# Seven block products (Strassen's scheme) instead of eight in the second layer of an attention and two-layer kernel, in tiles of 768 tokens

## What is computed

```python
def _moe_ref(x, w_in, w_out, s, b):
    h = x @ w_in
    r = np.maximum(h, 0.0)
    g = s * (r * r) + b
    return (g @ w_out).astype(np.float32)

def _moe2_ref(x, w_in, w_out):
    h = x @ w_in
    g = h - np.tanh(h)
    return (g @ w_out).astype(np.float32)
```

## Time and profile before

| | |
|---|---|
| median of 3 runs | 911.38 us (910.88 to 911.38) |
| span of the profiled execution (its own time isn't listed beside it) | 909.3 us |
| TensorE busy | 895.9 us, 6100 matmuls |
| VectorE busy | 501.7 us |
| ScalarE busy | 425.0 us |
| GpSimd busy | 279.4 us |
| mean granted TensorE clock | 0.998 |

### The profile page before, as it was taken

The page is one execution under the profiler, slowest core; times in us unless marked ns, Lnnn a source line. Parts: engine busy times, 40 slices in busy tenths (PEclk is TensorE's granted clock), DMA queues, the critical chain, the costliest instruction groups (busy, mean ns, idle before and its releaser), DMA issues.

```text
span 909.3 us, 15682 instructions
## 1 busy us (share of the span) xinstructions
PE 895.9 (99%) x6100; PEld 846.0 (93%) x6100; DVE 501.7 (55%) x635; ACT 425.0 (47%) x1060; POOL 279.4 (31%) x280
## 2 busy tenths in 40 slices
PE   6999999999999999999999999999999999999998
PEld 6789999999999999999999999999999999999997
DVE  5658599989999999982104632323323323322322
ACT  2899585566546754446457722322323223222221
POOL 6568474966497653534222000000000000000000
PEclk9999999999999999999999999999999999999999
DMA  8962453343344223002225400200200100100101
GB/s 217 274 236 55 127 146 85 91 121 85 97 114 115 62 61 78 19 2 65 66 77 181 165 1 1 70 1 1 70 1 22 49 1 1 35 1 1 35 1 35
DMA packets 48333, 65.15 MB, mean 72 GB/s; under 512 B 18246, under 2 KB 30084, under 8 KB 48260
## 3 DMA queue, kind: packets, MB, share of 16 engines
q1 hardware_dynamic: 45865, 62.42, 24.8%
q10 hardware_dynamic: 2395, 1.74, 0.8%
HBM read 54.71 MB, written 9.44 MB: 71 GB/s over the span
## 4 chain that ended last, share of the span: by engine, by line
PE 95%; ACT 2%; DMA 1%; DVE 1%; issue 1%; SPq 1%; ACTq 0%; DVEq 0%
PE acc L1918 22%; PE hid L1937 22%; PE hid L1890 21%; PE acc L1955 21%; PE pa L1848 1%; PE pa L1815 1%; DMA dkey<-in_k_dram 1%; PE pa L1832 1%; PE pa L1690 1%; PE pa L1861 1%; PE acc L1967 0%; PE hid L1898 0%; SPq L867 0%; PE hid L1796 0%; PE pa L1753 0%
## 5 line engine op out<-in xcount | busy, mean ns | idle before, releaser
L1057 POOL TENSOR_TENSOR gl<-relu,gh 128x288 fp32r<-128x288 f32 x128 | 128.6, 1008 | 185.9 <-PE acc L1918 129.5
L1361 DVE TENSOR_TENSOR gdif<-hid,tanh 128x384 f32<-128x384 f32 x96 | 53.5, 558 | 184.4 <-ACT tanh L1638 184.2
L1918 PE MATMUL acc<-gh,wbh 128*128 128x288 f32 (+1 forms) x512 | 154.6, 302 | 0.0
L1890 PE MATMUL hid<-xh,wah 128*128 128x288 f32 x512 | 153.5, 301 | 0.3 <-ACT relu L1597 0.2
L1918 PE MATMUL acc<-gl,wbh 128*128 128x288 f32 (+1 forms) x512 | 151.5, 296 | 0.0
L1918 PE MATMUL acc<-gh,wbl 128*128 128x288 f32 (+1 forms) x512 | 151.1, 295 | 0.0
L1890 PE MATMUL hid<-xh,wal 128*128 128x288 f32 x512 | 150.4, 295 | 0.0
L1890 PE MATMUL hid<-xl,wah 128*128 128x288 f32 x484 | 142.0, 294 | 0.0
L1638 ACT ACTIVATE tanh<-hid 128x384 f32<-128x384 f32 x96 | 47.2, 491 | 186.3 <-PE hid L1937 186.3
L1937 PE MATMUL hid<-x2h,wal 128*128 128x384 f32 x384 | 129.0, 336 | 0.0
L1937 PE MATMUL hid<-x2h,wah 128*128 128x384 f32 x384 | 128.9, 336 | 0.0
(11 more groups left out here) (162 smaller groups left out, 1549.9 us busy)
## 6 DMA issues: line engine op xcount, KB each, us to landing
wa_raw<-in_moe_w_in_dram SPq DMA_DIRECT2D x8, 1024.0 KB, 7.8
wb_raw<-in_moe_w_out_dram SPq DMA_DIRECT2D x8, 1024.0 KB, 6.3
kl<-in_k_dram SPq DMA_DIRECT2D x23, 240.0 KB
vl<-in_v_dram SPq DMA_DIRECT2D x23, 240.0 KB
...
x2raw<-x2T SPq DMA_DIRECT2D x6, 768.0 KB, 4.5
...
```

Source lines behind the costliest of these rows:

```text
L1057: g.tensor_tensor(out=gl[:, turn % LRING1, 0:NS], in0=relu[:, f % 2, :], in1=gh[:, turn % GRING1, 0:NS].bitcast(F32), op=ALU.subtract).the ...
L1361: ve.tensor_tensor(gdif[:, f % 2, :], hid[:, f % 2, 0:N2], tanh[:, f % 2, :], ALU.subtract).then_inc(s_dif, 1)
L1890: one = pe.matmul(dst, w[:, d, cols], x[:, j % XRING, d, :], start=i == 0, stop=i == 3 * KT - 1)
L1918: one = pe.matmul(acc[:, d, n], w[:, f, cols], g[:, turn % ring, n], start=(f == 0 and p == 0), stop=(f == FT - 1 and p == 2))
```

## The change

The tile becomes 768 tokens, in two halves of 384, and there are three. The hidden blocks are taken in pairs (`QUADS` = 8). For a pair, w_in is four blocks (two halves of the 512 inputs by two hidden blocks) and x2 is four blocks (two halves of the inputs by two halves of the tokens), and the four blocks of the hidden result are made from seven products of sums of these, not from eight plain ones (Winograd's form of Strassen's scheme). One pair in one tile is a step; there are 24. In a step:

- `product` p1, p6, p2, p7, p4, p5, p3: six matmuls of 384 columns each. p1 and p2 add up in bank 0 of `hid`, p7 and p4 in bank 1, p5 and p3 in bank 0.
- `copy1` (ScalarE) takes p1 out before p2 is added; VectorE forms `u2` = p6 + p1, `u3` = p7 + u2, `c21`, `c22` and `c12`, each from one PSUM bank and one SBUF tile. Then tanh, difference, high and low part for each of the four blocks of 128 by 384. Of these the low parts and the last three differences read two SBUF tiles.
- `out2`: the output of the step before in six chunks (row blocks of 128 tokens) of six matmuls of 512 columns, one behind nearly each product, into the four banks of `acc` and the two of `pa`.

The sums of the weight blocks are made once in place (`w2_sums`, VectorE, four instructions of 256 columns for each pair), then split: ScalarE `w2a_high` and GpSimd `w2a_low`, one instruction of 128 x 1792 each, 8 pairs. w_out doesn't stay: in each step 512 KB of it are loaded again into a ring of two (`load_w2b`), split by ScalarE and GpSimd (`w2b_low`, two instructions of 512 columns). x2 has 14 operands of 384 columns for a tile (7 block sums, two input halves); GpSimd makes the sums t1, t3, t2, t4 and the low parts of two of the seven, VectorE the other low parts; they replace those of the tile before product by product. The last three output blocks of layer one are moved between the first products of layer two.

```diff
-N2 = 384
+N2 = 768
 TILES2 = TOKENS // N2
-LAG2, GRING2 = 3, 4
+HALF2 = N2 // 2
+QUADS = FT // 2
+BLOCK2 = N2 // P
...
+PRODUCTS = {"p1": (A11, B11, 0, True), "p6": (S2, T2, 1, True), "p2": (A12, B21, 0, False),
+            "p7": (S3, T3, 1, True), "p4": (A22, T4, 1, False), "p5": (S1, T1, 0, True), "p3": (S4, B22, 0, False)}
...
+        o.add("SP", 2.4, (3, 2 * q), ("load_w2a", q), after, kbytes=512)
+        o.add("DVE", 1.8, (2, q), ("w2_sums", q), [("load_w2a", q)])
+        o.add("ACT", 1.65, (2, q), ("w2a_high", q), [("w2_sums", q)])
+        o.add("POOL", 4.7, (2, q), ("w2a_low", q), [("w2a_high", q)])
...
+        o.add("SP", 0.6, (3, 2 * n + 1), ("load_w2b", n), after, kbytes=512)
+        o.add("ACT", 1.25, (2, n), ("w2b_high", n), [("load_w2b", n)])
+        o.add("POOL", 2.9, (2, n), ("w2b_low", n), [("w2b_high", n)])
...
+        order = ["p1", outs[0], "p6", outs[1], "p2", "p7", outs[2], "p4", outs[3], "p5", outs[4], "p3", outs[5]]
...
+            elif kind == "w2a_low":
+                q, = key
+                g.wait_ge(s_w2ah, q + 1)
+                g.tensor_tensor(out=wql[q][:, :, :, :], in0=wq_raw[q][:, :, :, :], in1=wqh[q][:, :, :, :].bitcast(F32),
+                                op=ALU.subtract).then_inc(s_w2al, 1)
...
+            elif kind == "u3":
...
+                ve.wait_ge(s_product["p7"], n + 1)
+                ve.tensor_tensor(sum22[:, :], hid[:, 1, 0:HALF2], sum12[n % 2][:, :], ALU.add).then_inc(s_u3, 1)
...
+            elif kind == "c22":
...
+                ve.wait_ge(s_product["p5"], n + 1)
+                ve.tensor_tensor(sum22[:, :], hid[:, 0, 0:HALF2], sum22[:, :], ALU.add).then_inc(s_c22, 1)
...
+                ve.wait_ge(s_product["p3"], n + 1)
+                ve.tensor_tensor(u, hid[:, 0, 0:HALF2], u, ALU.add).then_inc(s_c12, 1)
...
+                if name == "p1":
+                    if n:
+                        pe.wait_ge(s_c12, n)
...
+                elif name == "p6":
+                    if n:
+                        pe.wait_ge(s_c21, n)
...
+                elif name == "p2":
+                    pe.wait_ge(s_copy1, n + 1)
+                elif name == "p7":
+                    pe.wait_ge(s_u2, n + 1)
+                elif name == "p4":
+                    pe.wait_ge(s_u3, n + 1)
+                elif name == "p5":
+                    pe.wait_ge(s_dif, 4 * n + 1)
+                elif name == "p3":
+                    pe.wait_ge(s_c22, n + 1)
+                for kk in range(2):
+                    for p, (wt, xt) in enumerate(((wqh[q], x2h), (wqh[q], x2l), (wql[q], x2h))):
+                        one = pe.matmul(hid[:, r, 0:HALF2], wt[:, w, kk, :], xt[:, x, kk, :],
+                                        start=fresh and kk == 0 and p == 0, stop=kk == 1 and p == 2,
+                                        skip_group_check=not fresh)
+                one.then_inc(s_product[name], 1)
...
+                for f in range(2):
+                    slot = n % 2 * 2 + f
+                    for p, (w, g) in enumerate(((w2bh, g2h), (w2bl, g2h), (w2bh, g2l))):
+                        one = pe.matmul(out_bank(i), g[:, n % 2, f, i * P:(i + 1) * P], w[:, slot, :],
+                                        start=(q == 0 and f == 0 and p == 0), stop=(q == QUADS - 1 and f == 1 and p == 2))
+                one.then_inc(s_used2, 1)
```

More of the change, by code:

```diff
@@ new lines, in plan @@
+    for q in range(QUADS):
+        after = [("hidden1", last, 7)] if q < 2 else [("hidden1", last, FT - 1)] if q < 4 else [("output1", last, FT - 1)]
+        if q == QUADS - 1:
+            after.append(("store1", last))
+        o.add("SP", 2.4, (3, 2 * q), ("load_w2a", q), after, kbytes=512)
+        o.add("DVE", 1.8, (2, q), ("w2_sums", q), [("load_w2a", q)])
+        o.add("ACT", 1.65, (2, q), ("w2a_high", q), [("w2_sums", q)])
+        o.add("POOL", 4.7, (2, q), ("w2a_low", q), [("w2a_high", q)])
@@ new lines, in build @@
+    o_ring = o_wbh
+    o_quads = [o_wah, o_wal, o_wah + quad, o_wal + quad] + [o_ring + 4 * 8 * DM + quad * i for i in range(3)]
+    o_g2 = o_x
+    o_quads.append(o_g2 + 4 * 4 * 4 * HALF2 * 2 // 2)
+    o_x2 = o_quads[-1] + quad
+    o_inter = o_x2 + 4 * 2 * 7 * 2 * HALF2
+    o_raw0 = o_inter + 5 * unit
+    o_raw1 = o_quads[6] + quad
+    assert o_raw1 + 4 * unit <= o_x and o_raw0 + 4 * unit <= nc.sbuf_usable_end and o_x2 >= o_att
+    wqh = [place(f"wqh{i}", [P, 7, 2, P], F32R, o_quads[i])[0] for i in range(QUADS)]
@@ new lines, in build @@
+    tanh11, _ = place("tanh11", [P, HALF2], F32, o_inter + 3 * unit)
+    tanh, _ = place("tanh", [P, HALF2], F32, o_inter + 4 * unit)
+    odd12, _ = place("odd12", [P, HALF2], F32, o_wal + 2 * quad + 4 * DM)
+    sum12 = (even12, odd12)
+    ostage = [place(f"ostage{i}", [P, DM], F32, o)[0]
+              for i, o in enumerate((o_wah + 2 * quad, o_wah + 2 * quad + 4 * DM, o_wal + 2 * quad))]
+    assert o_wal + 2 * quad + 4 * DM + unit <= o_wbh and o_wah + 2 * quad + 8 * DM <= o_wal
+    raw0, _ = place("x2raw0", [P, 2, N2], F32, o_raw0)
@@ new lines, in build, with high2_count, wait_low2, x2_raw @@
+    raw1, _ = place("x2raw1", [P, 2, N2], F32, o_raw1)
+    raw_first, _ = place("x2raw_first", [P, 2, N2], F32, o_inter)
+    def high2_count(j, kk, x):
+        return 14 * j + splits(j).index((kk, x)) + 1
+    def wait_low2(e, j, kk, x):
+        mine = [one for one in splits(j) if low2_maker(one[1]) == low2_maker(x)]
+        e.wait_ge(s_x2pl if low2_maker(x) == "POOL" else s_x2vl, j * len(mine) + mine.index((kk, x)) + 1)
+    def x2_raw(j, kk):
+        t = raw0 if kk == 0 else raw1 if j else raw_first
+        return [[t[:, k, h * HALF2:(h + 1) * HALF2] for h in range(2)] for k in range(2)]
@@ L637, in build, with x2_t1, x2_source @@
+    def x2_t1(j, kk):
+        return ostage[1 + kk][:, 0:HALF2] if j else tanh[:, :]
+    def x2_source(j, kk, x):
+        (r11, r12), (r21, r22) = x2_raw(j, kk)
+        return {B11: r11, B21: r21, B22: r22, T1: x2_t1(j, kk), T2: r11, T3: r12, T4: r21}[x]
     acc = nc.alloc_psum_tensor("acc", [P, 4, 512], F32)
@@ L842, in rows_of, with stage2, stage_uses @@
         return stores
-    def stored_count(j, i):
-        return sum(len(rows_of(one, i)) for one in range(j + 1))
+    def stage2(j, i):
+        return ostage_last[:, i - STAGES2, :] if j == TILES2 - 1 and i >= STAGES2 else ostage[i % STAGES2][:, :]
+    def stage_uses(j, i):
+        return (BLOCK2 * j + i) // STAGES2
     def store_rows(e, j, i):
         for rows, row, pattern in rows_of(j, i):
-            e.dma_start(dram(out, row * DM, pattern), ostage[rows, i, :]).then_inc(s_out[i], 16)
+            e.dma_start(dram(out, row * DM, pattern), stage2(j, i)[rows, :]).then_inc(s_out[i % STAGES2], 16)
     def store_half(e, half):
-        rows, row, pattern = rows_of(TILES2 - 1, 2)[half]
-        e.dma_start(dram(out, row * DM, pattern), ostage[rows, 2, :]).then_inc(s_out[2], 16)
+        j, i = TILES2 - 1, BLOCK2 - 1
+        rows, row, pattern = rows_of(j, i)[half]
+        e.dma_start(dram(out, row * DM, pattern), stage2(j, i)[rows, :]).then_inc(s_out[i % STAGES2], 16)
     def sync_program(sp):
@@ L1889, in tensor_program @@
                             pe.wait_ge(s_x0l, d + 1)
-                    one = pe.matmul(dst, w[:, d, cols], x[:, j % XRING, d, :], start=i == 0, stop=i == 3 * KT - 1)
+                    one = pe.matmul(dst, w[:, group, d, cols], x[:, j % XRING, d, :], start=i == 0, stop=i == 3 * KT - 1)
                 if f or not j:
@@ L1897, in tensor_program @@
                     wait_xlow(pe, j, d)
[L1898 removed]
+                    one = pe.matmul(hid[:, 0, 0:NS], wah[:, 0, d, 0:P], xl[:, j % XRING, d, :], start=False, stop=d == KT - 1)
                 one.then_inc(s_h, 1)
```

572 lines of the change are left out of this document (360 added, 212 removed).

## The result

The changed kernel takes **907.96 us** (median of 4 runs, 906.39 to 908.10) against 911.38: a ratio of 0.9966 with a 95% interval of 0.9953 to 0.9978. It is faster by 3.4 us where I forecast 9.1. The profiled execution has a span of 904.2 us against 909.3 (-5.1); the spans of the other three runs were 905.7, 905.8 and 905.9, so the profiled one flatters the change by 1.6, and the rest of the difference to the median is the 2.2 us around the span, about as before. The other three also had a lower mean granted clock, 0.989 to 0.991 against 0.994, so part of the 1.6 may be more time at the lower clock; no trace of them shows where.

What follows compares the result with a forecast made beforehand. TensorE, busy 895.9 of 909.3 us, was taken to bound the kernel. Terms -25.0 + 1.5 + 12 + 2.4 = -9.1 gave a 900.2 us span, 902.3 us with 2.1 carried over to the median; range 887 to 913.

Steps and rivals of the forecast that it cites:

- -25.0 for 144 matmuls: Layer two on TensorE: 1008 matmuls of 384 columns instead of 1152, at 0.1734 us each, -25.0 us.
- +1.5 for the two bare gaps of step 0: Step 0: p3 and the next p1 wait for VectorE's sums with nothing between, 2 x 0.76 = +1.5 us.
- the lock: SBUF port pair shared by VectorE and GpSimd: a two-SBUF-operand VectorE instruction can stand for one whole GpSimd instruction.
- +12 for GpSimd's six long instructions: Steps 0 to 2: six 4.07 us low-part instructions each block VectorE about 2.0 us; +12 us, ends 0 and 24.4.
- +0 for the clock: Where TensorE stands several us at the long instructions, its clock may fall; 0.8 us of work lost, no separate case.
- +0 for shorter groups: TensorE's groups of six matmuls with their own waits cost nothing, from 18 matmuls in 4.09 us.
- +2.4 for the boundaries: At two tile boundaries, splitting x2 makes c22 and c12 late: 2 x 1.2 = +2.4 us, ends 0 and 2 x 3.
- +0 for loads, SP's queue and GpSimd's short instructions in a step: Loads land a step early unless SP's queue is blocked; GpSimd's 512-column instructions meet only VectorE's PSUM-reading sums: 0.
- +2.1 from span to median: The earlier kernel's median lies 2.1 us above its profiled span; carried over from 900.2 to 902.3 us.
- hidden: Rival: GpSimd's long instructions meet VectorE's PSUM reads and waits for data, so 888.4 us (884 to 893); chance 0.25.
- the lock in every step: Slower rival: late output weights make GpSimd's 512-column instructions block VectorE in all 24 steps, +19, 921 us; chance 0.11.

Runs made afterwards that it cites:

- the best at 890.95: Against the changed kernel: weights' low parts on VectorE, step 0 and step 1 reordered, later weight sums and low parts placed where VectorE idled; 890.95 us (0.9782).

## Why the prediction was right or wrong

- **-25.0 for 144 matmuls**: right, products at 1.04.
- **+1.5 for the two bare gaps of step 0**: right; with the lock nearly gone they measured 0.8 + 0.7.
- **+12 for GpSimd's six long instructions**: the mechanism, its place, the 4.07 us and the waits (13.5 us by the sum with the bare gaps, 11.4 measured) were right. Two sizes inside were off and cancel, which is luck. A blocked instruction stood 2.9 us too long on average (17.7 us in six), not half of 4.07: in five of six cases one with two SBUF operands came up within 1.4 us of the start of GpSimd's. And not every us of that reached TensorE, as I had assumed: of the 17.7, TensorE waited for 9.9 at most.
- **+0 for the clock ("in the range and no case of its own")**: a term that I had put at nothing. It fell twice and cost an estimated 3.3 us. The long instructions and the clock together are 13.8 to 14.8 us by the run that took them away, where the sum had 12.
- **+0 for a start behind a wait**: not in the sum either; at most 1.5 us.
- **+0 for shorter groups ("shorter groups cost nothing")**: this is, with the clock, the step that failed. I had taken it from 18 matmuls of 512 columns that stood together; behind a change of shape a group of six takes 1.389 instead of 1.368. With the products behind it, that is 0.15 us in a step, 3.3 in all. Why the starts are slower stays open.
- **+2.4 for the boundaries**: 0.8.
- **+0 for loads, SP's queue and GpSimd's short instructions in a step**: right for the loads and SP's queue, and for the short instructions from step 3 on, where undisturbed steps took 15.64. Not in step 1: there the two sums of x2 held VectorE up by 0.7 and 0.8 us while TensorE waited. I had not counted them among the blocking ones.
- **+2.1 from span to median**: it was 3.8, since the profiled run was the fastest of four. That 1.7 is chance of which run was profiled, and no step of the sum.

In sum: transition +2.7 over the forecast (16.2 against 13.5: waits -2.1, clock +3.3, slow starts +1.5), chunks +3.3, boundaries -1.6, layer one -0.6, and 1.7 from the profiled run to the median make 5.5 of the 5.7 us between 902.3 and 907.96. The two terms put at nothing, clock and chunks, are 6.6, more than the whole miss; the waits and the boundaries, forecast too high, hid part of it. Of the rivals, "hidden" (888.4) did not come, since the long instructions met VectorE each time; only kernels without them come near it, the best at 890.95. Nor did the lock in every step. The Trainium skill (SBUF — State Buffer, Who interferes with whom) calls the lock exclusive and held for the whole instruction; the rows above agree, with GpSimd instructions of 4 us, a VectorE one of 2.02 the other way, and the two PSUM reads at 515 us that went through.
